# Attention, SoLU block, hard-swish block: who splits the first block's weights in the first batch, and in what order the engines take the work around it

## The reference

```
# 1: attention in chunks of 32 queries, 8 heads of width 64, 8 memory keys in front
scores = scale * q_c @ k_full.T;  scores -= max;  a = exp(scores)
a /= sum(a) + 1e-9;               out = a @ v_full
# 2: SoLU block
h = x @ w_in                      # 512 -> 1024
sm = softmax(h);  solu = h * sm
ln = (solu - mean) / sqrt(var + 1e-6) * g_ln
x2 = ln @ w_out                   # 1024 -> 512
# 3: hard-swish block
h = x2 @ w_in2                    # 512 -> 2048
out = (h * clip(h + 3, 0, 6) / 6) @ w_out2
```

## Time and profile before

| | |
|---|---|
| median of 3 runs | 943.51 us (942.12 to 944.47) |
| the profiled execution's own time | 945.21 us |
| its span in the profile | 943.4 us, 17258 instructions |
| busy share PE, DVE, ACT, POOL | 96%, 73%, 50%, 28% |
| start of the first, second, third, fourth hidden product | 35.92, 46.91, 61.81, 90.39 us |

### The profile page before, as it was taken

One profiled execution on the slowest core, in us unless ns is written; L12 is line 12 of the kernel. 1 busy time (PEld: TensorE's weight loads), 2 busy tenths in 40 slices (PEclk: granted clock), 3 DMA queues, 4 the chain that ended last, 5 costly groups with the idle time before them and its releaser, 6 DMA issues.

```text
span 943.4 us, 17258 instructions
## 1 busy us (share of the span) xinstructions
PE 907.4 (96%) x6200; PEld 811.4 (86%) x6200; DVE 684.1 (73%) x1095; ACT 471.7 (50%) x1092; POOL 267.2 (28%) x317
## 2 busy tenths in 40 slices
PE   8887999999999999999999999999899999999998
PEld 7666888989888888888978888888689999999997
DVE  3898688878777777857585555555688978878783
ACT  4555465555556565625575555455544333333320
POOL 5452165554422353551103332233420000000000
PEclk8988999999999999999999999999999999999999
DMA  8723336566754376468453233333967434344441
GB/s 191 157 56 62 93 77 174 155 178 178 217 129 133 109 195 163 151 210 331 148 216 139 104 133 133 133 133 114 359 257 282 140 105 157 108 139 130 136 138 45
DMA packets 146907, 146.46 MB, mean 155 GB/s; under 512 B 96936, under 2 KB 107176, under 8 KB 145832
## 3 DMA queue, kind: packets, MB, share of 16 engines
q1 hardware_dynamic: 134328, 100.55, 36.8%
q0 software_dynamic: 7920, 38.94, 11.6%
q10 hardware_dynamic: 4608, 6.29, 1.9%
HBM read 90.05 MB, written 55.71 MB: 154 GB/s over the span
## 4 chain that ended last, share of the span: by engine, by line
PE 75%; DVE 13%; DMA 6%; ACT 3%; issue 2%; POOL 1%; SPq 1%; ACTq 0%; DVEq 0%; POOLq 0%
PE banks L858 22%; PE banks L1042 21%; PE banks L901 20%; PE banks L812 3%; DMA g_scratch<-part 3%; PE banks L781 2%; DVE prob L1301 2%; PE banks L838 2%; PE banks L825 2%; DVE gs L1277 2%; PE banks L849 2%; DVE gs_raw L1457 1%; DMA k_in<-in_k_dram 1%; DMA x_mix_scratch<-x_mix 1%; DMA xs_raw<-x_mix_scratch 1%
## 5 line engine op out<-in xcount | busy, mean ns | idle before, releaser
L1042 PE MATMUL banks<-vs,gs 128*128 128x256 f32 x2016 | 243.3, 283 | 2.5 <-DVE o_stage L1491 1.5
L1042 PEld LDWEIGHTS banks<-vs,gs 128*128 128x128 f32 x2016 | 242.3, 192 | 3.5 <-DVE o_stage L1491 1.7
L901 PE MATMUL banks<-xs,ws 128*128 128x512 f32 x1008 | 233.2, 392 | 6.1 <-ACT part L1139 4.3
L901 PEld LDWEIGHTS banks<-xs,ws 128*128 128x128 f32 x1008 | 189.2, 189 | 48.6 <-issue 4.6
L1237 ACT CAST gs<-gs_raw 128x1792 fp32r<-128x1792 f32 x48 | 81.4, 1695 | 132.2 <-DVE gs_raw L1457 132.2
L858 PE MATMUL banks<-y_t,w_out 128*128 128x384 f32 x768 | 140.9, 338 | 1.3 <-DVE y_t L1277 1.3
L858 PE MATMUL banks<-w_in,x_t 128*128 128x512 f32 x552 | 133.8, 398 | 1.1 <-DVE solu L1331 1.1
L858 PEld LDWEIGHTS banks<-y_t,w_out 128*128 128x128 f32 x768 | 132.1, 188 | 2.2 <-issue 1.7
L858 PEld LDWEIGHTS banks<-w_in,x_t 128*128 128x128 f32 x552 | 103.6, 191 | 23.3 <-DVE solu L1331 1.4
L1090 ACT ACTIVATE prob<-score,small 96x128 f32<-96x128 f32 x256 | 99.2, 392 | 19.2 <-DVE small L1290 19.2
L1457 DVE TENSOR_TENSOR gs_raw<-gs_raw 128x256 f32<-128x256 f32 x192 | 81.4, 424 | 30.4 <-DMA gs_raw<-g_scratch 25.5
(11 more groups left out here) (88 smaller groups left out, 1064.9 us busy)
## 6 DMA issues: line engine op xcount, KB each, us to landing
g_scratch<-part SPq DMA_DIRECT2D x96, 256.0 KB, 2.1
gs_raw<-g_scratch SPq DMA_DIRECT2D x45, 512.0 KB, 3.9
q_in<-in_q_dram SPq DMA_DIRECT2D x32, 192.0 KB, 4.0
x_scratch<-x_out ACTq DMA_DIRECT2D x32, 192.0 KB, 1.9
out_dram<-o_stage SPq DMA_DIRECT2D x12, 512.0 KB, 5.7
k_in<-in_k_dram SPq DMA_DIRECT2D x24, 240.0 KB
v_in<-in_v_dram SPq DMA_DIRECT2D x24, 240.0 KB
v_split_scratch<-v_split POOLq DMA_DIRECT2D x3, 1792.0 KB, 7.8
```

Source lines behind the costliest of these rows:

```text
L901: mm = pe.matmul(ps, ws[:, W_OF[i], a, kc, :], xs[g][X_OF[i]][:, m, kc, :], start=(fresh and x == 0), stop=(x == len(passes) - 1), skip_gr ...
L1042: mm = pe.matmul(m_ps[i][:, s, :], gs[x][:, a, G_OF[i], s * P:(s + 1) * P], vs[p][:, m, V_OF[i], :], start=(p == 0 and s == 0 and y == 0), ...
```

## The change

GpSimd waits until the first k has arrived before it requests pieces 0 and 1 and g_ln. Pieces 2 to 7 get a place of their own (`w_later`, in the room of `y_t1`, which is not yet in use), so a request waits only for the landing of the piece two before it. GpSimd runs through all 8 pieces in a row, ahead of `normalise`, and only scales and casts them (`high_weights`); ScalarE casts none. VectorE makes all 8 low halves (`low_weights`), pieces 0 and 1 in step 1, 2 and 3 in step 2, 4 in step 3, 5 and 6 in step 4, 7 in step 5. In the first batch VectorE's `solu_and_stats` moves from the end of its step to the next one, behind `max_scores` and the low half of the weights; `low_x` and `high_x` go between the two halves of the probabilities; TensorE's `attend` goes ahead of `hidden`; the six dummy matmuls of step 4 fall away.

```diff
-        w_raw = at("w_raw", 184, [P, 2, PIECE], F32)
+        w_first = at("w_first", 184, [P, 2, PIECE], F32)
+        w_later = at("w_later", 112, [P, 6, PIECE], F32)
...
+        def w_piece(p):
+            return w_first[:, p, :] if p < 2 else w_later[:, p - 2, :]
+        def w_split_at(p, a):
+            if p < WP1:
+                return w_in[:, a, p, :]
+            c = 2 * (p - WP1)
+            return w_out[:, a, c:c + 2, :].rearrange("p c n -> p (c n)")
...
 # gpsimd
-            def split_weights(p):
-                pool.wait_ge(w_raw_here[s], 16 * (p // 2 + 1))
...
-                nc.gpsimd.tensor_copy(hi, raw).then_inc(w_hi_done, 1)
-                pool.wait_ge(w_hi_done, p + 1)
-                nc.gpsimd.tensor_tensor(lo, raw, hi.bitcast(F32), ALU.subtract).then_inc(w_lo_done, 1)
-                pool.wait_ge(w_lo_done, p + 1)
-                if p + 2 < 2 * WP1:
-                    load_weights(p + 2)
+            def high_weights(p):
+                pool.wait_ge(w_raw_here[p % 2], 16 * (p // 2 + 1))
+                raw = w_piece(p)
+                if p + 2 < 2 * WP1:
+                    load_weights(p + 2)
+                if p >= WP1:
+                    c = 2 * (p - WP1)
                     pool.wait_ge(g_ln_here, 16)
                     for x in range(2):
                         last = nc.gpsimd.tensor_scalar(...)
                     last.then_inc(w_scaled, 1)
                     pool.wait_ge(w_scaled, p - WP1 + 1)
+                nc.gpsimd.tensor_copy(w_split_at(p, HI), raw).then_inc(w_hi_done, 1)
...
-            load_weights(0)
-            load_weights(1)
-            pool.dma_start(g_ln, ...)
...                       # masks
             pool.wait_ge(mask_ready, 1)
+            pool.wait_ge(k_in_here[0], kv_here(0, 0))
+            load_weights(0)
+            load_weights(1)
+            pool.dma_start(g_ln, ...)
+            for p in range(2 * WP1):
+                high_weights(p)
...
-                    # the calls of split_weights in steps 0 to 6
 # tensor
                         if kk < TPG:
                             turn_early_qk(kk)
-                        keep_busy(6)
+                            keep_busy(6)
...
+                    if first and w["before"]:
+                        attend(0, kk - 2, kk == 2)
                     if w["mm1"]:
                         hidden(i, u, (ii + 1) % 2, first)
...
-                    if w["before"]:
+                    if w["before"] and not first:
                         attend(...)
 # scalar
-            def exp_scores(n):
+            def exp_scores(n, between=None):
                 for half in range(2):
+                    if half and between:
+                        between()
...
-                        nc.scalar.copy(w_in[:, HI, 0, :], w_raw[:, 0, :]).then_inc(w_hi_done, 1)
...
+                    if first and w["before"]:
+                        exp_scores(n, lambda: high_x(n - 1, (kk - 2) % TPG, (kk - 2) // TPG % 2))
 # vector
+            def low_weights(p):
+                dve.wait_ge(w_hi_done, p + 1)
+                low(w_split_at(p, LO), w_piece(p), w_split_at(p, HI)).then_inc(w_lo_done, 1)
...
                     if w["own"]:
                         max_scores(n, {0: 2, 1: 0}.get(kk, 1), first and kk == 1)
-                    if first and kk == 0:
-                        dve.wait_ge(w_hi_done, 1)
-                        low(w_in[:, LO, 0, :], w_raw[:, 0, :], w_in[:, HI, 0, :]).then_inc(w_lo_done, 1)
+                    if first:
+                        for p in {1: (0, 1), 2: (2, 3), 3: (4,), 4: (5, 6), 5: (7,)}.get(kk, ()):
+                            low_weights(p)
+                    if first and kk > TPG:
+                        solu_and_stats(kk - TPG - 1, kk == TPG + 1)
                     if w["turn"]:
                         low_ln(turned_tile(i, u), u, ii if u == 0 else (ii + 1) % 2)
-                    if w["own"]:
+                    if first and w["before"]:
+                        norm_probs(n, lambda: low_x(n - 1, (kk - 2) % TPG, (kk - 2) // TPG % 2))
+                    elif w["own"]:
                         norm_probs(n)
                     if w["mm1"]:
                         max_hidden(MPG * (i - 1) + u)
-                    if w["before"]:
+                    if w["before"] and not first:
                         low_x(n - 1, (kk - 2) % TPG, (kk - 2) // TPG % 2)
-                    if w["mm1"]:
-                        solu_and_stats(MPG * (i - 1) + u, first and u == 0)
+                    if w["mm1"] and not first:
+                        solu_and_stats(MPG * (i - 1) + u, False)
```

More of the change, by code:

```diff
@@ L523, in load_weights @@
             def load_weights(p):
-                s = p % 2
                 if p < WP1:
                     src = moe_w_in.rearrange("(c p) n -> p c n", p=P)[:, p, :]
-                    dst = w_raw[:, s, :]
+                    dst = w_piece(p)
                 else:
                     src = moe_w_out.rearrange("(c p) n -> p c n", p=P)[:, 2 * (p - WP1):2 * (p - WP1) + 2, :]
-                    dst = w_raw[:, s, :].rearrange("p (c n) -> p c n", c=2)
-                pool.dma_start(dst, src).then_inc(w_raw_here[s], 16)
-            def split_weights(p):
-                s = p % 2
-                pool.wait_ge(w_raw_here[s], 16 * (p // 2 + 1))
[L538 to L541, removed]
+                    dst = w_piece(p).rearrange("p (c n) -> p c n", c=2)
+                pool.dma_start(dst, src).then_inc(w_raw_here[p % 2], 16)
+            def high_weights(p):
[4 more added lines that the diff above has]
+                if p >= WP1:
                     c = 2 * (p - WP1)
-                    hi, lo = (w_out[:, a, c:c + 2, :].rearrange("p c n -> p (c n)") for a in (HI, LO))
                     pool.wait_ge(g_ln_here, 16)
@@ L581, in _ @@
             pool.wait_ge(mask_ready, 1)
+            pool.wait_ge(k_in_here[0], kv_here(0, 0))
+            load_weights(0)
+            load_weights(1)
+            with nc.allow_non_contiguous_dma(reason="one vector, once"):
+                pool.dma_start(g_ln, moe_g_ln.rearrange("(c p) -> p c", p=P)).then_inc(g_ln_here, 16)
+            for p in range(2 * WP1):
+                high_weights(p)
             def normalise(m, u, slot_new):
@@ L966, in batch @@
                         project(i, 3, ii, last and ii)
-                    if w["before"]:
-                        attend(b if kk > 1 else b - 1, (kk - 2) % TILES, first and kk == 2)
+                    if w["before"] and not first:
+                        attend(b if kk > 1 else b - 1, (kk - 2) % TILES, False)
                     if first and kk == TILES - 1:
@@ L1163, in batch @@
                         copy_qk(kk, early_ps)
-                    if first and kk == 0:
-                        act.wait_ge(w_raw_here[0], 16)
-                        nc.scalar.copy(w_in[:, HI, 0, :], w_raw[:, 0, :]).then_inc(w_hi_done, 1)
                     if w["before"]:
@@ L1291, in max_scores, with norm_probs @@
                                             ).then_inc(smax_done, 1)
-            def norm_probs(n):
+            def norm_probs(n, between=None):
                 for half in range(2):
+                    if half and between:
+                        between()
                     hs = slice(HB * half, HB * (half + 1))
```

2 lines of the change are left out of this document (removed).

## The result

| | before | after |
|---|---|---|
| median | 943.51 us (942.12 to 945.74, 5 runs) | 951.38 us (949.28 to 956.26, 5 runs) |
| ratio | | 1.0086, 95% interval 1.0057 to 1.0115 |
| the profiled execution's own time | 945.21 us | 954.93 us |
| its span | 943.4 us | 953.1 us |

The account below looks back on a forecast made before the run. VectorE's path to the fourth hidden product was taken as the bound, TensorE being full afterwards. 34 + 5 locks + 14.4 + 13.3 + 22.3 = 89.0, plus 3 of clock, gave 92.0, 1.6 later: 945.1 us, range 939.5 to 950.5.

Parts of the forecast that it names:

- the mark: Start of the fourth hidden product on TensorE, 90.39 us before; forecast at 92.0, 1.6 us later, moving the kernel equally.
- The locks: VectorE and GpSimd excluding each other on SBUF work: 12.9 us before; GpSimd's remaining casts and scalings would cost VectorE 5.
- the 1.8 named: Sign of being right: VectorE's two-operand L1301, stretched before, never takes above 1.8 us.
- a named sign of being wrong: VectorE's low halves of weights taking 1.23 us even beside GpSimd's casts.
- the row at 62.82, named for PSUM operands: VectorE's operations with a PSUM operand, at 62.82 and 65.45, were not stretched though GpSimd worked at 63.76.
- Requests: Weight pieces 0 and 1 requested at 6 to 7 us; second k's turn about 11.5, tile 0's exponentials 1.4 us sooner.
- slower rival: Late solu_done and slow clock ahead of second and third hidden products: mark at 96.0, 949.1 us; late weights add 1.5; chance 0.38.
- First hidden product: On TensorE, start at 34 us without locks, 35.92 before; sign of being right: 38 to 41.
- Distances: Between hidden products: first to second 14.4 us (11.0 before), second to third 13.3 (14.9), third to fourth 22.3 (28.6).
- 3 of clock: TensorE's slow clock after new waits and without step 4's dummies, up to the mark: 3 us, bounds 1 and 7.
- The gain from third to fourth: Third to fourth hidden product 6.3 us shorter, from locks, clock and maxima no longer waiting behind the sums.
- faster rival: GpSimd's casts run under VectorE's maxima and ScalarE waits: locks 1, clock 1.5, mark at 86.5, 939.6 us; chance 0.22.

Follow-up runs that it names:

- dummies off: The kernel before without the six dummy matmuls of step 4 of the first batch, nothing else: 948.79 us, ratio 1.0066.
- dummies back: The changed kernel with the six dummy matmuls of step 4 given back: 946.49 us, ratio 1.0048 to the kernel before.
- dummies in 7: The changed kernel with six more dummies in step 7 (22 instead of 16), none in step 4: 946.05 us, ratio 1.0030 to the kernel before.
- shift experiment: The kernel before with 40 more dummy matmuls (56 instead of 16) in step 7 of the first batch: 967.16 us, ratio 1.0255.
- the second profile: The changed kernel run again as it is, on another chip: 950.55 us, ratio 1.0077 to the kernel before.
- weights only: The changed kernel with the old order of VectorE, ScalarE and TensorE and the dummies of step 4: 937.25 us, ratio 0.9931 to the kernel before.
- order only: The kernel before with the new order of VectorE, ScalarE and TensorE, weights and dummies as before: 946.15 us, ratio 1.0027.

## Why the prediction was off

**The step that failed** is the first one: "From about 90 us on TensorE is busy 10.00 of 10 us, and the remaining 850 us do not change", with its sequel that what the mark gains or loses, the kernel gains or loses. The row behind it covers 100 to 110 us, and none looked at the hand-over. The mark was forecast 1.6 us later and came 2.8 and 0.3 later. The hand-over at 399 to 443 us lost 3.6 and 3.2 us more, and dummies off, dummies back and dummies in 7 put that on the six dummies that the change removes. I had priced them for their clock alone. The shift experiment breaks the same step in a second way, with 17.5 us more between the mark and the last scores for an edit that touches no instruction of the loop.

**The locks** were right in size: 4.9 and 3.8 us for 5 on VectorE, and L1300's longest was 1.38 us, under the 1.8 named. But a named sign of being wrong came half true: the two low halves that began at 38.56 took 2.35 us together beside a scaling, unstretched, and that pair of scalings took 4.25 us in place of 1.36. The price was mutual. As I read it, VectorE works nearly without pause here and so seldom lost the start to GpSimd; six of eight low halves took 1.21 to 1.23 us, and GpSimd's scalings paid 8 x (1.27 - 0.68) = 4.7 us. The casts were over at 43.7, not 35, partly for that. One reading of the prediction is too wide: the engines do not exclude each other on all operations that read SBUF alone. The reduction of the scores (L1290) reads SBUF alone, with one operand, and kept its 0.68 us beside GpSimd's scalings in the kernel before:

```profile
64.85 0.68 DVE L1290 TENSOR_REDUCE small<-score 96x4 f32<-96x512 f32 x1
```

```profile
64.93 1.35 POOL L546 TENSOR_SCALAR w_raw<-w_raw,small 128x512 f32<-128x512 f32 x2
```

And the row at 62.82, named for PSUM operands, ended at 63.50, before the GpSimd instruction set beside it began (63.76).

**Requests** went out at 6.73, inside 6 to 7, and the second k's turn came at 11.9, for 11.5. The exponentials of tile 0 began 1.0 us sooner, for 1.4. VectorE waited 1.8 us for the cast of piece 3, which the forecast had only in its slower rival (1.5).

**First hidden product** forecast at 38 to 41: 39.06, and 36.60 in the second profile. The range left out how far two executions of one program differ by then, mostly in VectorE's wait for a cast and in its locks.

**Distances.** First to second 15.2 (14.4 forecast), second to third 14.8 (13.3), third to fourth 24.1 (22.3): 54.1 us for 50.0 and 3 of clock. The waits behind `solu` are the ones described, 4.43 and 2.26 us. So the mechanism held and the clock was some 1 us dearer. What I did not see is the alternative: with the sums in their old place the distances are 10.0, 15.1 and 20.7. The gain from third to fourth, which I put partly to the new order of the maxima, came from either part by itself: 28.6 us before, 23.5 with weights only, 25.2 with order only. With the new split and the dummies the late sums took 2.9 us of it back (23.6 against 20.7). Each of these distances is from one profile.

**The rivals.** The slower one named the median nearly (949.1), and its place, the waits ahead of the second and third hidden products. But in the profiles its price was not paid: it wanted the mark at 96.0, and it came at 93.18 and 90.73. The right side was reached in part by another cause. The faster rival needed locks of 1 us; they cost 4.9 and 3.8.

**What stays open.** That the count of TensorE's instructions ahead decides the hand-over is shown; that it does so by the place of the code, and a fetch which meets SyncE's requests, is a reading: the fetch falls into the requests in the three profiles without the dummies, where they take 2.5 to 2.7 us, and outside them in the other ten, where they take 1.39 or 1.40. But one packet that is 5.2% of 16 engines in 1.5 us, 1.2 us of one engine, doesn't by itself explain loads that land 3.4 to 4.3 us later. The shift had 40.7 us too, so another count doesn't always cost; by this reading it costs where it puts the fetch on the requests. From the third stage's first product to the end the changed kernel took 2.8 and 1.4 us more than before, the other variants from 503.6 to 509.9 us (507.1 before). In the three profiles without the six dummies the granted clock of the first 20 us of that stage was 0.91, in the ten others 1.00, which by itself is worth 0.09 x 20 = 1.8 us (an estimate); the wait for `xs` ahead of it is part of the price of the hand-over. For the rest of the spread I have no cause. The changed kernel with the dummies, at 1.0048 and 1.0030, still carries the late sums, though its profiles end only 1.4 to 1.6 us above before's. Places are read from one profile a kernel, and the kernel before alone ran from 937.09 to 947.47 us in 29 runs on one chip; its four runs below 940 had a mean clock of 0.989 to 0.992, most of the others 0.981 to 0.988. So the shares of a few us at the mark are less sure than the medians.

## What to carry to other kernels

When an edit adds or removes instructions ahead of a loop or of a tight hand-over, count them: the same stage can become 3 us longer, or each return to a loop's start cost 5 to 8 us, without any change in its own code, and a control with the count restored tells that apart. Price the order of work by the consumer that frees a shared buffer (`solu_done` here), not by the engine's total: with the new split, moving the sums behind the next maxima cost 10 to 11 us, where moving the weights gained 6 to 7 (with the old split the whole new order cost 0.27%, some 2.5 us). Test each part of a bundled change by itself, and in both settings; here a gain of 0.7% lay hidden under two losses, and the price of the order depended on the split.

## What the runs showed of the hardware

- Code fetches can bound TensorE: 40 dummies (160 records) ahead of a loop gave 15 fetches in 200 us where there had been none, and 13.6 us of waits for "issue" at the loop's two returns, the longest 5.3.
- 24 records fewer on TensorE, in three profiles of two kernels: SyncE's three requests at the hand-over took 2.5 to 2.7 us in place of 1.39 or 1.40, their 512 KB loads landed after 8.2 to 9.0 us in place of 4.7 or 4.8, and the 1 MB store behind them after 10.1 to 11.8 us in place of 6.5 to 8.5 in the ten others.
- Where VectorE issued two-operand SBUF work back to back, GpSimd paid: its 128x512 scaling took 1.27 us on average in place of 0.69 (1.00 to 1.27 in the seven other profiles of the new split), while VectorE's 128x1024 subtraction stayed at 1.21 to 1.23 in six of eight, and in all eight of the second profile.
